# An expert kernel: a shorter wait before the second tile's load, and the split of the next weights placed behind the tiles

## The reference

```python
# 1. attention (2 batches, 8 heads, 768 tokens, head size 64), sink and window mask
x = attn_out.transpose(0, 2, 1, 3).reshape(1536, 512)
# 2. dense gated layer, width 1536
x = (silu(x @ w_gate) * (x @ w_val)) @ w_out
# 3. routed layer: 8 experts, width 1024; each token goes to one expert
do_compute = x @ w_skip > 0
out = x.copy()
xc = x[do_compute]
logits = xc @ w_gate2
e_idx = argmax(logits);  gate_w = softmax(logits)[e_idx]
for e in range(8):
    h = maximum(xc[e_idx == e] @ w1[e], 0)
    y[e_idx == e] = gate_w * (h @ w2[e])
out[do_compute] = xc + y
```

## Time and profile before

| | us |
|---|---|
| median of 3 executions | 578.85 |
| lowest and highest of them | 576.34, 579.18 |
| the profiled execution | 577.65 |
| its span in the profile | 576.1 |
| TensorE busy | 551.4 (96%) |
| VectorE (DVE) busy | 242.9 (42%) |
| ScalarE (ACT) busy | 181.2 (31%) |
| GpSimd (POOL) busy | 95.1 (17%) |

### The profile page before, as it was taken

How to read it: one execution, slowest core, us unless ns; L and a number is a source line. 1 busy time by engine, 2 the same in 40 slices (tenths; PEclk the granted TensorE clock), 3 DMA queues, 4 the chain that set the end, 5 groups by cost and what they waited for, 6 DMA issues and landing times.

```text
span 576.1 us, 10759 instructions
## 1 busy us (share of the span) xinstructions
PE 551.4 (96%) x3837; PEld 465.8 (81%) x3837; DVE 242.9 (42%) x686; ACT 181.2 (31%) x421; POOL 95.1 (17%) x137
## 2 busy tenths in 40 slices
PE   7899999999999999999999999999869999999994
PEld 5677777888888888888888888887759988999993
DVE  6777772323223323332323436543714144255311
ACT  4667772111101111111224335231313133244110
POOL 2233457211111110000000010101200101111111
PEclk9899999999999999999999999999989999999997
DMA  7888622100111111000081114651645786845111
GB/s 215 207 275 247 184 98 65 69 24 31 55 55 55 55 55 55 0 0 1 0 304 54 44 58 165 233 200 55 202 162 223 283 329 234 338 166 202 55 38 36
DMA packets 29591, 73.84 MB, mean 128 GB/s; under 512 B 2832, under 2 KB 15120, under 8 KB 25456
## 3 DMA queue, kind: packets, MB, share of 16 engines
q1 hardware_dynamic: 26592, 63.61, 32.4%
q0 software_dynamic: 2960, 9.73, 5.0%
HBM read 62.03 MB, written 11.29 MB: 127 GB/s over the span
## 4 chain that ended last, share of the span: by engine, by line
PE 83%; DMA 7%; DVE 4%; issue 2%; SPq 1%; ACT 1%; POOL 0%; POOLq 0%; DVEq 0%; ACTq 0%
PE bank L1279 11%; PE bank L1281 11%; PE bank L1283 11%; PE bank L1484 7%; PE bank L1356 6%; PE bank L1360 6%; PE bank L1358 6%; DMA w_raw<-w 4%; PE bank L1265 4%; PE bank L1242 3%; PE bank L1496 3%; PE bank L1498 3%; PE bank L1497 3%; PE bank L1221 3%; PE bank L1376 2%
## 5 line engine op out<-in xcount | busy, mean ns | idle before, releaser
L1279 PE MATMUL bank<-x_hi,w_hi 128*128 128x512 f32 x288 | 112.2, 390 | 0.5 <-issue 0.5
L1283 PE MATMUL bank<-x_hi,w_lo 128*128 128x512 f32 x288 | 112.1, 389 | 0.0
L1281 PE MATMUL bank<-x_lo,w_hi 128*128 128x512 f32 x288 | 112.0, 389 | 0.0
L1484 PEld LDWEIGHTS bank<-xgT,w_sb 128*128 128x128 f32 x704 | 80.2, 192 | 1.8 <-issue 1.1
L1484 PE MATMUL bank<-xgT,w_sb 128*128 128x128 f32 x704 | 80.5, 275 | 0.8 <-ACT xgT L801 0.8
L997 DVE TENSOR_TENSOR sig<-sig,bank 128x512 f32<-128x512 f32 x36 | 24.8, 688 | 127.3 <-ACT sig L703 127.3
L703 ACT ACTIVATE sig<-bank 128x512 f32<-128x512 f32 x36 | 21.5, 598 | 159.7 <-PE bank L1283 159.7
L1279 PEld LDWEIGHTS bank<-x_hi,w_hi 128*128 128x128 f32 x288 | 54.1, 188 | 12.1 <-issue 0.9
L1283 PEld LDWEIGHTS bank<-x_hi,w_lo 128*128 128x128 f32 x288 | 54.1, 188 | 11.4
L1281 PEld LDWEIGHTS bank<-x_lo,w_hi 128*128 128x128 f32 x288 | 54.1, 188 | 11.1
L1087 DVE TENSOR_TENSOR w_lo<-w_raw,w_hi 128x1024 fp32r<-128x1024 f32 x32 | 37.3, 1219 | 39.2 <-ACT w_hi L763 39.1
(11 more groups left out here) (169 smaller groups left out, 744.5 us busy)
## 6 DMA issues: line engine op xcount, KB each, us to landing
w_raw<-w SPq DMA_DIRECT2D x16, 1024.0 KB, 7.5
w_sb<-w SPq DMA_DIRECT2D x16, 1024.0 KB, 6.3
w_raw<-w_gv SPq DMA_DIRECT2D x12, 512.0 KB, 3.6
va_sb<-v_long SPq DMA_DIRECT2D x10, 512.0 KB, 3.6
vb_sb<-v_tail SPq DMA_DIRECT2D x10, 320.0 KB, 4.5
xg<-expert_rows POOLq DMA_DIRECT2D x12, 257.0 KB, 3.0
q_sb<-qT SPq DMA_DIRECT2D x12, 256.0 KB, 5.1
k_sb<-kT SPq DMA_DIRECT2D x12, 256.0 KB, 6.2
```

The lines of the kernel that those rows point to most:

```text
L1279: nc.tensor.matmul(ps[:, :], w_hi[:, u, a, k, :], x_hi[:, k, tok], start=(k == 0), stop=False)
L1281: nc.tensor.matmul(ps[:, :], w_hi[:, u, a, k, :], x_lo[:, k, tok], start=False, stop=False)
L1283: last = nc.tensor.matmul(ps[:, :], w_lo[:, u, a, k, :], x_hi[:, k, tok], start=False, stop=(k == KD - 1))
L1484: last = nc.tensor.matmul(ps, w1_sb[u][:, k, fc], xgT[:, k * P:k * P + P], start=(k == 0), stop=(k == KD - 1))
```

## The change

SP's second store of empty rows gets a semaphore of its own, second_padded. POOL waits for this one (and, as before, for the first) ahead of the load of the rows of tile 1. The wait for the other six stands between the wait for xres and the load of the number of tiles, ahead of POOL's loop. On ACT and on DVE the split of w2 of expert e + 1 stands behind the loop over the tiles of expert e, where it stood ahead of it.

```diff
-        first_padded = sem("first_padded")
+        first_padded, second_padded = sem("first_padded"), sem("second_padded")
@@ SP @@
                 sp.dma_start(expert_rows[bass.ds(filled + e * CAP, P), :], pad[:, :]
-                             ).then_inc(padded if e else first_padded, 16)
+                             ).then_inc((first_padded, second_padded)[e] if e < 2 else padded, 16)
@@ POOL @@
             pool.wait_ge(first_padded, 16)
             pool.dma_start(xres[:, 0, :], expert_rows[0:P, :]).then_inc(first_kept, 16)
             pool.wait_ge(routed, 1)
-            pool.wait_ge(padded, 16 * (E - 1))
+            pool.wait_ge(second_padded, 16)
             load_rows(1)
             pool.wait_ge(first_kept, 16)
+            pool.wait_ge(padded, 16 * (E - 2))
             total = pool.value_load(first_i[0:1, E:E + 1], min_val=E, max_val=MAXT - 2)
@@ ACT @@
                     begin, end = tiles(a, e, end if u else None)
+                    expert_tiles(begin, end)
                     split_ahead(e + 1, u, begin)
-                    expert_tiles(begin, end)
```

## The result

| | before | after |
|---|---|---|
| median of the runs, us | 578.18 (6 runs, 576.34 to 579.18) | 569.08 (6 runs, 567.21 to 569.32) |
| the profiled execution, us | 577.65 | 567.21 |
| its span, us | 576.1 | 565.6 |
| g0's start to g1's start, us | 20.01 | 14.25 |
| g1's start to g10's start, us | 120.04 | 117.66 |

The ratio of after to before is 0.984, with a 95% interval of 0.9817 to 0.9863: the kernel became 9.1 us faster in the medians. 569.2 was forecast. In two later measurements, each beside the kernel before, the changed kernel was 7.2 and 7.7 us faster.

The account below looks back on a forecast made before the run. TensorE, busy 96% of the span, was taken as the bound, with time to win only where it stops or runs slow. 6.1 + 2.4 = 8.5 us off the profiled 577.65 gave 569.2 us, range 567.0 to 574.0.

Parts of the forecast that it names:

- Part A: POOL's shorter wait before loading tile 1's rows: the second tile's products start 6.1 us earlier, of at most 6.94.
- Part B: The w2 split behind the tiles on ACT and DVE: stalls at the fourth and fifth tiles go, 2.4 us.
- the old 1.71 us from release to start: POOL's delay before the load of tile 1's rows, kept from the old trace; bounds 0.6 us earlier to 0 later.
- I take 4.1: Time in us for the load of tile 1's rows, taken from xres; least 2.97, most 6.5.
- The estimate of 2.6 us: The skill's fit for the load of tile 1's rows, about 2.0 us plus bytes over 436 GB/s.
- the slow stretch: TensorE's lowered clock, 0.77, after its wait for tile 1's rows; costs 1.66 us and was to go.
- Rival 1: Tile 1's rows come only a little earlier, the clock may fall: part A 2.0 us, time 573.2; chance 0.15.
- Rival 2: Moving the splits moves their stalls instead of removing them: part A alone, 571.6 us; chance 0.12.
- Rival 3: Slower than before: raw w2 becomes the bound at one-tile experts, 580.6 us or more; chance 0.04.
- threshold: Raw w2's second half must land by 15.8 us into a one-tile expert, 14.7 us after its issue.
- Rival 4: POOL is held by something the old wait hid, part A does little: 575.2 us; 0.07 including mixtures under 2.9 us.
- The moved wait: POOL's later wait for six stores: tile 2's rows still land in time, 2 us to spare, cost nothing.

Follow-up runs that it names:

- B alone: Kernel before, with only ACT's and DVE's splits moved behind the tiles and POOL still waiting for all eight stores: 575.42 us, ratio 0.9958.
- ACT's split ahead: Changed kernel with ACT's split put back ahead of the tiles, DVE's left behind them: 587.27 us, ratio 1.0164 against the kernel before.

## Why the prediction was right

**The sum.** Part A was 6.1 us and measured 5.8 in the first profile, 5.4 and 2.8 in the two others. Part B was 2.4 and measured 2.38. The sum was 8.5; the first profile gives 8.14, the medians 9.1, 7.2 and 7.7, all within the range. That 569.08 came so close to 569.2 is partly luck: 569.2 was reckoned down from the profiled execution, and from the median before (578.18) the same 8.5 us give 569.7.

**Part A.** Two errors nearly cancelled, which is luck. "From there I take the old 1.71 us from release to start" was too long: L613 started 1.17 us after the xres instruction (413.47 + 0.58 to 415.22), because the 0.50 us that its register load took in the earlier trace rows do not follow that instruction. This is just under the prediction's own bound of 0.6 us earlier. (Against g0's start, the forecast of 417.6 to 418.2 is 3.3 to 3.8 us; it was 3.18, 3.64 and 3.70.) "I take 4.1" for the load was too short: 5.07, 6.01 and 4.92 us in the three profiles. xres, from which I took it, ran beside the last four stores of empty rows, with nothing ahead of it on POOL's queue. The load, in the first profile, ran beside the last three stores and beside xres itself, issued 1.75 us before it. The runs take these apart: with the stores and xres ahead of it the load took 4.3 to 6.0 us in six executions, with the stores and xres behind it 3.9 and 4.2, with xres ahead and no stores 3.76, with xres behind and no stores 3.6. So the row for the price was well chosen, and the transfer that it left out was POOL's own. The estimate of 2.6 us that the Trainium skill (DMA: Bandwidth & Descriptors, Anatomy of one DMA) would give was never seen in this place. Its other rule (Issuing engines are not separate DMA queues), that a transfer from POOL shares the engines with SP's, agrees with the runs with and without the stores: behind xres the load took 0.5 to 2.3 us more beside them.

**The clock.** "So the slow stretch goes too" was right in two of three profiles. Its size, 1.66 us, was measured apart as 1.64. What was missing is that the load's time varies from one execution to the next, and that the clock can go with it: behind waits of up to 1.25 us it was at 1.00, behind the one of 2.29 us it was not, and then another 1.6 us went.

**Rival 1** was a form of the same event rather than another course. It had the load at 6.5 us and g1 18.0 us after g0; one execution of six had 6.01 and 17.26. For a single execution that is about the 0.15 it was given; a median takes more than one. **Rival 2** was wrong; B alone gave its 2.4 us and the whole 2.38. **Rival 3** has its mechanism (late raw data do stall) but not its case: made to land 8 us later on purpose, it cost 1.4 us in one place. Its threshold was about 1 us too generous, by one place. The reading behind it has an error that changed nothing: 463.9 and 478.6 are not the two halves of one expert's raw w2 but the second halves of those of experts 3 and 4. **Rival 4** did not happen.

**The moved wait and the splits.** The last six empty rows were indeed no hindrance in the changed kernel, and there was more to spare than the 2 us of the prediction. The load of tile 2's rows started at 421.88, 9.8 us after g0's start where 12.4 was the forecast. What released it in the first profile was DVE's copy of tile 1's rows (L1150); the last store had landed 2 us before. It took 6.7 us, and TensorE wanted the rows 4.9 us after they had landed (6.3 and 4.7 in the other two profiles). The splits came 8.31 us into the last tile of an expert (447.67 against g2's start at 439.36), forecast 8.43, and ACT waited for no raw data.

## What to carry to other kernels

When a wait is shortened, price what now comes last on the waiting engine (here its own indirect store and one more load), and the transfers that run beside the released one, the engine's own included. A step that only looks ahead, such as preparing the next weights, belongs behind the work that is due now, on every engine that shares it; left ahead on one of two, it cost 18 us here. And a gap of TensorE that shrinks to about a microsecond in one profile may be longer in the next, with a slow clock behind it: look at more than one execution.

## What was not expected of the hardware

- Behind a wait of 2.29 us the clock was at 0.77 over the next 7.57 us, much as behind 5.01 us, and behind one of 2.84 us at 0.81 over 7.31 us; waits of 1.25, 1.17 and 1.15 us left it at 1.00. But waits do not tell everything. In one execution (ACT's split ahead) it was 0.81 over g0 with no wait longer than 0.96 us near by, and L1485 took 9.04 us instead of 7.41. In another (the changed kernel, second profile) it was 0.72 over 402 to 408 us with none over 0.38. No run was made to explain these two.
- The same load of 257 KB took 2.97 us alone, 3.6 to 3.8 with xres near by, 3.9 and 4.2 with stores beside it and xres behind it, 4.3 to 6.0 with stores beside it and xres ahead of it.
- POOL's copy of an index column (128 x 1) took 0.20 us at five tiles of the changed kernel's first profile. At the six where it fell beside DVE's subtractions of two SBUF operands (L1088) it took 0.35 to 1.19 us. It costs nothing here. The Trainium skill (SBUF — State Buffer, SBUF: two separate sides) has DVE and GpSimd share a port pair as an exclusive lock, also for a DVE operation with two SBUF inputs against a GpSimd operation that reads SBUF. The trace agrees: none of the copies took longer than one of the subtractions (1.22 us). The start of a DMA in the same stretch took its usual 0.55 us. From the timelines of POOL and DVE of the changed kernel:

```profile
462.51 0.55 POOL L613 DMA_DIRECT2D xg<-expert_rows  x1 [6.61 <-issue]
463.06 1.19 POOL L618 CAST idx_out<-xres 128x1 int32 x1
```

```profile
461.84 4.63 DVE L1088 TENSOR_TENSOR w_lo<-w_raw,w_hi 128x1024 fp32r<-128x1024 f32 x4 [0.41 <-ACT w_hi L764]
```
